# Delta-rule attention, a dense MoE and a routed MoE in one kernel: the first chunk pair solved chunk by chunk, GpSimd and the third pair's steps at other places

## The reference, cut to what matters

```python
B, H, S, D = 4, 8, 768, 48
k_n = k / (norm(k) + 1e-06)
for t in range(S):
    y[:, :, t] = einsum('bhd,bhde->bhe', q[:, :, t], state)
    v_old = einsum('bhde,bhd->bhe', state, k_n[:, :, t])
    state = state + beta[:, :, t] * einsum('bhd,bhe->bhde', k_n[:, :, t], v[:, :, t] - v_old)
h = maximum(maximum(x @ w1, x @ w2), x @ w3)     # x: 3072 x 384, w: 384 x 768
x = h @ w_out
# routed: top 2 of 8 by x @ w_gate + log1p(exp(x @ w_noise)) * noise, experts 384 -> 1024 -> 384
```

## Time and profile before

| | us |
|---|---|
| median of 3 runs | 1048.62 |
| profiled execution | 1045.29 |
| its span | 1043.5 |
| TensorE busy | 1004.7 (96%) |
| VectorE busy | 723.3 (69%) |
| ScalarE busy | 475.9 (46%) |
| GpSimd busy | 214.7 (21%) |

### The profile page before, as it was taken

One profiled execution on the slowest core, in us unless ns is written; L12 is line 12 of the kernel. 1 busy time (PEld: TensorE's weight loads), 2 busy tenths in 40 slices (PEclk: granted clock), 3 DMA queues, 4 the chain that ended last, 5 costly groups with the idle time before them and its releaser, 6 DMA issues.

```text
span 1043.5 us, 25843 instructions
## 1 busy us (share of the span) xinstructions
PE 1004.7 (96%) x10445; PEld 934.1 (90%) x10445; DVE 723.3 (69%) x1655; ACT 475.9 (46%) x708; POOL 214.7 (21%) x244
## 2 busy tenths in 40 slices
PE   7888998999999999999999999999999999999994
PEld 7877797889889889889899999999999999999994
DVE  6987545587577578543559776777677686776774
ACT  3622325324423523423254555556465465655553
POOL 0080083030021021031306212112211112212111
PEclk8899998999999999999999999999999999999998
DMA  9340140150160051116646536225252526535221
GB/s 331 91 110 2 37 109 2 56 151 2 42 158 9 17 129 24 28 62 221 199 154 205 161 63 181 49 45 161 45 160 46 167 39 173 167 68 146 42 35 23
DMA packets 71459, 102.04 MB, mean 98 GB/s; under 512 B 28624, under 2 KB 59856, under 8 KB 70992
## 3 DMA queue, kind: packets, MB, share of 16 engines
q1 hardware_dynamic: 59296, 78.51, 24.7%
q0 software_dynamic: 10992, 20.70, 10.4%
q10 hardware_dynamic: 1088, 1.65, 0.5%
HBM read 140.53 MB, written 29.51 MB: 163 GB/s over the span
## 4 chain that ended last, share of the span: by engine, by line
PE 83%; DVE 8%; ACT 3%; POOL 3%; issue 2%; POOLq 0%; DVEq 0%; ACTq 0%
PE ps L1641 40%; PE ps L1805 19%; PE ps L1689 6%; PE ps L1520 3%; PE ps L1816 2%; PE ps L1503 2%; PE ps L1705 2%; PE ps L1620 2%; DVE prod L1010 2%; DVE x L1014 2%; PE ps L1600 2%; POOL x L642 1%; PE ps L1610 1%; POOL pool_prod L639 1%; PE ps L1561 1%
## 5 line engine op out<-in xcount | busy, mean ns | idle before, releaser
L1641 PE MATMUL ps<-xr,wr_in 128*128 128x512 f32 x972 | 241.4, 402 | 1.1 <-DVE h L1104 0.5
L1641 PEld LDWEIGHTS ps<-xr,wr_in 128*128 128x128 f32 x972 | 181.4, 191 | 42.6 <-DVE wr_in L1097 0.9
L1641 PE MATMUL ps<-xbT,w1r 128*128 128x256 f32 x1728 | 211.6, 283 | 0.7
L1641 PEld LDWEIGHTS ps<-xbT,w1r 128*128 128x128 f32 x1728 | 209.7, 192 | 2.5 <-issue 2.5
L1805 PE MATMUL ps<-w2r,hbT 128*128 128x384 f32 x1152 | 205.9, 336 | 0.0
L1805 PEld LDWEIGHTS ps<-w2r,hbT 128*128 128x128 f32 x1152 | 198.9, 188 | 0.0
L670 POOL DMA_INDIRECT out_rows<-yb,idx x55 | 90.2, 1640 | 379.0 <-DVE yb L1322 289.6
L1134 DVE TENSOR_TENSOR w1r<-w1s,w1r 128x768 fp32r<-128x768 f32 x128 | 121.2, 957 | 18.7 <-ACT w1r L807 16.5
L823 ACT ACTIVATE hbT<-ps 128x512 fp32r<-128x512 f32 x96 | 57.4, 598 | 166.6 <-PE ps L1641 166.6
L807 ACT CAST w1r<-w1s 128x768 fp32r<-128x768 f32 x128 | 104.5, 828 | 24.3 <-DMA w1s<-in_we 24.3
L1134 DVE TENSOR_TENSOR w2r<-w2s,w2r 128x768 fp32r<-128x768 f32 x128 | 113.8, 951 | 1.8 <-ACT w2r L811 1.8
(11 more groups left out here) (216 smaller groups left out, 1139.4 us busy)
## 6 DMA issues: line engine op xcount, KB each, us to landing
w1s<-in_we SPq DMA_DIRECT2D x32, 1536.0 KB
w2s<-in_we SPq DMA_DIRECT2D x32, 1536.0 KB
xb<-rows SPq DMA_DIRECT2D x25, 402.0 KB, 3.9
kv_s<-in_kv SPq DMA_DIRECT2D x24, 384.0 KB, 3.5
k_s<-in_k SPq DMA_DIRECT2D x12, 512.0 KB, 3.8
joint<-in_q SPq DMA_DIRECT2D x24, 256.0 KB, 4.7
out_rows<-padrow SPq DMA_DIRECT2D x13, 384.0 KB, 4.3
w_in<-in_w_blocks SPq DMA_DIRECT2D x3, 1152.0 KB, 11.0
```

Of the source, the lines that this page charges most:

```text
L1641: mm = pe.matmul(dst, w, m, start=(opens and n == 0), stop=(closes and n == len(todo) - 1))
```

## The change

It has three parts.

1. **The first pair, chunk by chunk.** Low product, its copy, corner and solve blocks are made for chunk 0 first and for chunk 1 beside chunk 0's solution (`first_low`, `first_corner`, `first_solve`). k times q of chunk 0 is computed behind the gate fold, in other banks, and copied to SBUF by ScalarE. The first state is copied rather than added to zero. The diagonal blocks of chunk 1 are copied by ScalarE and VectorE in halves, and the off-diagonal blocks of the second pair go first to spare memory (`off_early`, in the tile `w_oT`) and are moved by GpSimd.
2. **GpSimd.** It does v's scaling and the masks of chunk 0, the low parts of weight blocks 0, 3 and 5 and of the output weights, and 12 and 20 inversion steps of pairs 1 and 2 instead of 16 and 24. Each has a wait that places it.
3. **Places.** Pair 1's low product goes from slot 9 to 11 of tile 0, with Gram 4 in slot 10 before it; pair 2's from slot 2 to 6 of tile 1, and all its steps by four. The second transpose of an inverse stands one slot after the first, and `solve_diagonals` one slot later, in all tiles. In tile 0 the third pair's blocks are transposed before r, and its norms are cut in three. The norms are one operation shorter for all pairs.

The diff, cut to its core:

```diff
-        POOL_STEPS = {1: 16, 2: 24}
+        POOL_STEPS = {1: 12, 2: 20}
-            return {1: H_BANKS, 2: H_BANKS, 3: D_BANKS}.get(c, E_BANKS)
+            return {1: H_BANKS, 2: H_BANKS, 3: D_BANKS, 4: D_BANKS}.get(c, E_BANKS)
-        START = {0: 8, 1: 1}
+        START = {0: 10, 1: 5}
...
-            tight = {"low": 1, "corner": 2, "gram0": 3, "gram1": 4, ...
+            tight = {"low": 1, "corner": 2, "gram0": 0, "diag0": 2, "gram1": 3, ...
...
                 if cp == 0:
+                    sp.wait_ge(p_rp, 1)
+                    load_columns(4)
                     sp.wait_ge(p_corner, 1)
                     sp.wait_ge(s_solve, 1)
                     load_q(1)
...
+            pool.wait_ge(s_half, 10)
+            pool.wait_ge(s_base, STEPS)
+            scaled_v(0)
+            pool.wait_ge(s_vn, 1)
+            first_pT(0)
+            weights_low(0)
+            zero_x(1)
+            pool.wait_ge(s_xz, 2)
+            first_pT(1)
+            pool.wait_ge(p_low, 1)
+            pool.wait_ge(s_off, 4)
+            nc.gpsimd.tensor_copy(off[:], off_early).then_inc(s_off_moved, 1)
+            pool_base(1)
+            pool.wait_ge(s_win, 3)
+            weights_low(3)
+            pool.wait_ge(s_base, base_before(2))
+            pool.wait_ge(s_win, 5)
+            weights_low(5)
...
@@ scalar @@
+            early_off_diagonals_of(2)
+            early_off_diagonals_of(3)
             weights_high()
+            first_k_q()
             out_weights_high()
-            low_times_inverse(0)
-            solve_diagonals(0)
-            corner(0)
-            off_diagonals_of(3)
-            off_diagonals_of(2)
+            first_low(0)
+            first_solve(0, 0)
+            first_solve(0, 1)
+            first_corner(0)
             roots(1)
+            first_low(1)
+            first_solve(1, 0)
+            first_solve(1, 1)
             u_out(0)
+            first_corner(1)
+            first_state()
...
                         if i == place(t, "low"):
                             low_times_inverse(cp)
+                        if i == place(t, "corner"):
                             solve_diagonals(cp)
-                        if i == place(t, "corner"):
                             corner(cp)
-                        if i == place(t, "gram0") and cp + 1 < CP:
+                        if i == place(t, "diag0") and cp + 1 < CP:
                             diagonals_of(c + 2)
...
@@ vector @@
+            half_diagonals()
             rows_of(0)
             norms(0)
+            norm_columns(0)
             base(0, 0, Q - 1)
             columns_of(0)
-            norm_columns(0)
-            scaled_v(0)
+            transposed_columns_of(0)
             rows_of(1)
-            corner_half()
-            pT_out(0)
-            norms(1)
-            weights_low(0)
-            state_out(0)
-            weights_low(1)
+            first_corner_half(0)
+            norms(1, (0,))
+            u_half(0)
+            first_corner_half(1)
+            norms(1, (1,))
+            first_state()
+            norms(1, (2,))
             scaled_v(1)
+            weights_low(1, (0, 1))
             r_out(1)
-            pT_out(1)
+            pT_out(1, (0,))
+            weights_low(1, (2,))
             u_half(1)
+            pT_out(1, (1,))
             norm_columns(1)
-            weights_low(2)
             state_out(1)
             y_half(1)
-            weights_low(3)
+            weights_low(2)
             x_low(0)
...
@@ tensor, gram(c) @@
-                if c >= 4:
+                if c >= 5:
                     pe.wait_ge(s_diag, c)
-                if c >= 4 and c % 2 == 0:
+                if c == 5 or c >= 6 and c % 2 == 0:
                     pe.wait_ge(s_corner, c // 2 * 2)
...
```

More of the change, by code:

```diff
@@ L721, in corner @@
                 act.wait_ge(s_solve, cp + 1)
-                for h_ in range(2 if cp else 1):
+                for h_ in range(2):
                     rows = slice(h_ * L, h_ * L + Q)
@@ L1072, in state_out @@
             def state_out(c):
+                first = C_BANKS if c > 1 else H_BANKS
                 dve.wait_ge(p_s, c + 1)
```

323 lines of the change are left out of this document (230 added, 93 removed).

## The result

The changed kernel took a median of 1060.82 us (1059.64 to 1061.75, 4 runs), the kernel before 1048.44 (1048.14 to 1052.35, 4 runs) on the same chip. The ratio is 1.0109, with a 95% interval of 1.0083 to 1.0135. The prediction was 1047.6 in a range of 1039.5 to 1055, with 0.16 on slower by over 0.5%: it was wrong, and the time lies outside its range. The profiled execution took 1059.64, its span is 1057.9 (before 1043.5).

What follows compares the result with a forecast made beforehand. TensorE was busy for 96% of the span, so only its waits could win. 8.0 + 1.2 - 5.3 - 4.6 + 1.7 made 1.0 us faster: span 1042.5, median 1047.6, range 1039.5 to 1055.

Steps and rivals of the forecast that it cites:

- Chain, +8.0: First pair of chunks, up to tile 0's x transposes: 8.0 us gained, between 5 and 10.
- q of chunk 1 at 52, product of 3.3 in full clock: First pair: q's load lands about 52 us, costing 1.5; k times state then takes 3.3 us.
- My lower bound of 5: Least gain for the first pair's chain, if GpSimd's masks are late and a half-clock pause occurs.
- Tile 0, +1.2: Tile 0: 5.2 us of present losses against new waits of 1.1 and 2.85, 1.2 gained.
- Tile 1, -5.3: Tile 1: present losses of 3.0 us become 8.3 (0.85, 4.3 and 3.15), 5.3 lost.
- Tiles 2 and 3, -4.6: Gram behind the corners waits 2.9 instead of 0.6 us in each tile, 4.6 lost.
- Tiles 4 and 5 have no Gram there: Later tiles: no Gram behind the corners, so no loss from the moved solve diagonals was counted.
- Clock, +1.7: Half-clock stretches after tiles 0 and 1's waits: two instead of three, 1.7 us each, 1.7 gained.
- Rival 2: Waits of 2.9 to 4.3 us in tiles 0 to 3 each bring half clock, 1.7 each: 1054.4; chance 0.13.
- Rival 3: First pair: GpSimd's masks and ScalarE's longer queue keep the chain as long within 3 us: 1052.6; chance 0.10.
- a price of some 0.9 on each weight piece of GpSimd: Three GpSimd weight pieces hold up VectorE's inversion steps by up to some 0.9 us each.

Runs made afterwards that it cites:

- experiment 13: The kernel before, unchanged, measured once more: ratio 0.9995; its profiled execution took 1052.4 us.
- experiment 1: Changed kernel plus 24 warming matmuls between chunk 0's outputs and k_state_and_q of chunk 1: ratio 1.0091.
- experiment 8: Experiment 2 plus 14 warming matmuls behind chunk 0's outputs, pair 2's steps at START 1 of tile 1, 24 on GpSimd, old spread: 1042.81 us, ratio 0.9938.
- experiment 10: Experiment 8 with START 2 instead of 1 in tile 1 and 21 instead of 24 steps on GpSimd: ratio 0.9942.
- experiment 11: Experiment 10 plus 12 warming matmuls before tile 1's low product and 16 before Gram 5 of tile 0: ratio 0.9921.
- experiment 16: Experiment 8 with 21 GpSimd steps, 28 warming matmuls before tile 1's low product and 16 before Gram 5 of tile 0: 1036.60 us, ratio 0.9930.
- experiment 2: Changed kernel with solve_diagonals and the inverse's second transpose back at their old slots in tiles 0 to 4: 1048.26 us, ratio 0.9975.
- experiment 12: The changed kernel itself, measured once more: ratio 1.0106.
- experiment 15: Changed kernel with only pair 2's steps at START 1 of tile 1, 24 on GpSimd, and their old spread: ratio 1.0065.
- after: The first profile of the changed kernel itself: profiled execution 1059.64 us.
- experiment 3: Changed kernel plus 38 warming matmuls before the first Gram of tiles 2 and 3: ratio 1.0087.
- experiment 6: Changed kernel plus 24 warming matmuls before the first Gram of tiles 2 and 3: ratio 1.0082.
- experiment 14: Changed kernel with solve_diagonals and the second transpose back at their old slots from tile 2 on only: ratio 1.0013.
- experiment 7: Kernel before plus 14 warming matmuls behind chunk 0's outputs and 18 before the low products of tiles 0 and 1: ratio 0.9968.
- experiment 5: Changed kernel with all places and inversion shares of the third part old, first pair and GpSimd's other work as changed: 1047.14 us, ratio 0.9966.
- experiment 9: Experiment 5 plus 14 warming matmuls behind chunk 0's outputs and 18 before the low products of tiles 0 and 1: 1043.58 us, ratio 0.9927.

## Why the prediction was wrong, step by step

The forecast span was 1042.5, the profiled one 1057.9. Of these 15.4 us the chain missed 6.6, tiles 1 to 3 with the clock's term 8.5, tile 4 2.6, and tile 0 was 2.3 better than forecast. Some 4 of the 15.4 are the small pauses in the tiles (experiment 13). Most waits were forecast in place and length; what was not is how much half clock would follow them.

**Chain, +8.0: the step "q of chunk 1 at 52, product of 3.3 in full clock" failed.** The order and the times to the state step were right. Measured were 1.4 and 5.7 us of gain in two profiles. Of the 6.6 missing in the first, 4.1 is half clock in product and u (6.24 and 3.18, against 3.28 and 2.07 in experiment 1), 0.7 the warming matmuls behind the product, in half clock too, and 1.8 q, at 53.80 instead of 52. Without half clock and a late fold the x transposes start at 65.2 to 67.0, a gain of 4.9 to 6.8 (experiments 8, 10, 11, 16 with warming behind the outputs, 2, 12, 15 without). My lower bound of 5 named "a pause in half clock" and gave it too little. The fold's weights, a second cause of delay, were in no bound.

**Tile 0, +1.2: right, too small.** Waits of 0.7 and 2.6 against 1.1 and 2.85. The gain was 3.5 and 3.7. In the first pair of profiles 1.6 is waits and some 1.2 the one half-clock stretch less; 0.7 isn't traced.

**Tile 1, -5.3: the sum right, a part of it by chance.** The waits grew by 5.7. Third low product 3.9 (4.3 predicted), h 0.9 (0.85), first output product 1.7 (3.15). The step that failed is the list of what waits: a state step for u's copy, 2.1, was not in it. ScalarE and TensorE of after:

```profile
208.21 0.62 ACT L917 CAST hT<-h 128x512 fp32r<-128x512 f32 x1 [10.66 <-DVE h L1276]
208.84 1.28 ACT L837 ACT_TABLE_LOAD   x1
...
210.52 0.58 ACT L907 COPY h<-ps 128x512 f32<-128x512 f32 x1
211.00 1.61 ACT L866 COPY joint<-ps 64x768 f32<-64x768 f32 x2
212.66 1.51 PE L1816 MATMUL ps<-joint,kv_s 64*48 64x48 f32 x58 [2.10 <-ACT joint L866]
```

Cast, the square root's table load and the root stand ahead of the copy and wait for VectorE, which transposes the third pair's blocks first. The earlier trace rows had the same 2.1 in tile 0 for the same reason; I had counted its going there and not its coming here.

**Tiles 2 and 3, -4.6: right** (2.86 twice, 2.9 predicted; experiment 2 gives them back). "Tiles 4 and 5 have no Gram there" was true and not enough: in tile 4 the copy of h stands behind the same two operations, and a product waits 1.4.

**Clock, +1.7: failed, with the chain's half clock the costliest step.** I took two half-clock stretches in the tiles after, against three. There were five, and nine in the second profile, against three and five of the kernel before. With the chain's it is eight and nine (27.3 and 30.7 us) against four and six. Three of them stand behind the late corners of tiles 2 and 3, and are absent where that wait is gone or filled (experiments 2, 3, 6, 14). Their price was mis-sized the other way: 7.7 us of span for 20.4 us between experiments 13 and 7, 3.4 for 10.2 in experiment 6, so 1.1 to 1.3 a stretch instead of 1.7. By the Trainium skill (TensorE: Matmul & The Clock Gate, Terms) half of the slow time is lost, as I had reckoned; the runs show a third and a little more, and at the corner of tile 1 in experiment 7 nothing, because ScalarE ended last there. In the tiles I was off by some 4 in the first pair of profiles (I had forecast a gain of 1.7, and two stretches more at 1.2 are a loss of 2.4) and by 6.5 in the second.

**Rivals.** Rival 2, half clock behind the long waits, is what happened: at three of the five places that it names in the first profile, at all five in the second. Its 1054.4 was still 6 too low, for it took the chain's 8.0 as won. I had given it 0.13 with the argument that the wait of 2.1 in tile 0 brought none. Experiment 13 shows the same wait in the same kernel with half clock behind it (132 to 136 us at 0.69). One execution had been read as a rule. Rival 3 did not occur by its mechanism: GpSimd's masks ran from 38.69 and 45.03, 2.4 each, and were there in time.

**Shared ports.** The Trainium skill (SBUF — State Buffer, Who interferes with whom) was cited for a price of some 0.9 on each weight piece of GpSimd. The page makes an exception that I left out: in VectorE's 2-port perf modes an instruction with one SBUF input excludes GpSimd too. In the trace of after the price is some 0.5 in all: the three pieces, from 72.06 to 74.99, lie mostly beside VectorE's work on PSUM, and only the first pair of inversion products behind it, at 74.40, took 0.94 where the later ones of some 130 elements keep 0.48. In experiment 1 a VectorE operation of 32 elements on two SBUF tiles took 1.04 at 47.03 and ended with a mask of GpSimd's, which ran from 45.63 to 47.98; it took 0.24 in after. Both agree with the rule.

**What is settled and what not.** Shown by putting back: the places cost some 15 us (experiment 5 against changed), of which 9.8 is solve_diagonals and the second transpose from tile 2 on (14) and 4.4 START 5 with its share of steps (15), each put back alone; chain and GpSimd's work are worth 3.6 together, not told apart from each other. Not settled: what decides whether a pause of 1.6 to 2.8 us is followed by half clock, and what the small pauses without a cause are.

## What to carry to other kernels

A wait of TensorE costs its length and, where the clock falls behind it, here a third of the slow time more, or nothing where another engine ends last; price both, and take from one profile neither that a wait of 2 us is harmless nor that it isn't. Before an operation is moved behind another on an in-order engine, list everything behind it there in every later tile, not only the step that it feeds. In every wait that warming matmuls filled whole the clock stayed at 1.00; that gains only if they are no longer than the wait, and if the time isn't lost again at the next one (experiments 7, 9 and 16). A list of them behind a load makes the load's delay the chain's.

## What the runs showed of the hardware

- Half clock after a pause is not a property of the program: the same chain with a pause of 1.6 to 1.9 us was followed by 10.2 us of it (after, 3, 6, 14), by none (2, 12) and by 3.4 (5). Gram 5's wait of 2.84 was followed by a stretch in 1 and 6 and by none in 3 and 14. At waits of 2.86 and more in the tiles (after, 1, 2, 3, 6, 8, 10, 12, 14, 15) there was always some.
- Warming matmuls of 128x128 took 0.12 us each in a row (2.94 for 24, 4.40 for 38).
- The kernel before ran in two groups beside experiments 10 to 13, 1047.4 to 1050.0 and 1052.1 to 1052.9, and at 1041.9 to 1047.5 on the chip of 14 to 16, with tiles of 80.6 instead of 82.2 us. The difference between two single profiles can hold 4 us that no edit made.
